# A tuned three-layer kernel: VectorE multiplies each row tile by w_skip, expert scores only of gathered early rows

## The chip, the cores and the metric

The kernel runs on one core of a Trainium2 chip. The metric is the device time of one execution in microseconds (us); the times shown are medians of several executions.

## The reference

Sparse attention over 4 batches of 8 heads (half local, half strided, 576 positions, head size 64), a dense layer pair (512 to 2048 to 512 with a clipped square between), and a mixture of 8 experts behind a skip decision. The last part is what the change touches; `x` holds 2304 rows of 512.

```python
    skip_score = x @ w_skip
    do_compute = skip_score > 0
    out = x.copy()
    xc = x[do_compute]
    logits = xc @ w_gate
    e_idx = np.argmax(logits, axis=1)
    gate_w = softmax(logits)[arange, e_idx]
    for e in range(E):
        mask = e_idx == e
        h = np.maximum(xc[mask] @ w1[e], 0.0)
        y[mask] = gate_w[mask, None] * (h @ w2[e])
    out[do_compute] = xc + y
```

With the inputs that are timed, the reference keeps 4 of the 2304 rows (numbers 11, 23, 1161 and 1177; experts 2, 2, 0 and 2). All others leave as they are.

## The kernel before

The 2304 rows are worked on in 6 chunks (`CHUNKS`) of 384 rows, each of 3 row tiles of 128. A chunk is 16 steps; in step s TensorE forms one 128-wide slice of the hidden layer (`hidden`, L1004, 12 matmuls: each factor is split in a high and a low part, three products of four slices) and adds the slice of two steps earlier to the three row tiles of the output (`output`, L1020, 9 matmuls). In between VectorE clips (L1367) and takes the maximum (L1370), ScalarE squares (L1625) and rounds (L1634), GpSimd forms the low part (L1748). `hidden(s)` waits for the maximum of step s-2; `output` comes two steps after its `hidden`.

All else is hung into 32 places of a chunk (`places_of_chunk`): even places lie, on TensorE, between `hidden` and `output` of a step, odd ones behind `output`; on VectorE even ones lie between clip and maximum, odd ones behind the maximum. Each engine works its own list of jobs in that order, so a job that waits holds everything behind it on its engine. The jobs:

- attention units, one in three places in chunks 2 and 3 (two late ones in chunk 1): `S` scores (PE L829; DVE mask and maximum L1139, L1143; POOL subtracts L1665), `X` exponentials (ACT L1514), `E` sums and reciprocals (DVE L1165 to L1170; POOL scales L1672), `P` transposes (PE L846, ACT L1524), `V` values (PE L865, ACT L1532, DVE L1175).
- `score_jobs(c)`, seven jobs for each chunk c, hung into places 6 to 17 of the chunk behind it: three `Y` (`turn_rows`, PE L875 transposes a row tile, ACT L1540 keeps it), two `Z` (`score_parts`, PE L886 multiplies by w_gate and w_skip), two `A` (`row_scores`, PE L895 adds up groups; DVE L1185 keeps 9 scores a row). For the last chunk they run only in the general part (`PLACES_AFTER`); its skip scores are products of VectorE (`last_skips`, L1312).
- early experts: when the rows of the first 4 chunks are scored, places 19 to 30 of chunk 4 rank all 1536 rows (`rank`, `count` PE L906), find the rows of the first two tiles of 32 slots, each of one expert (`choose` DVE L1259, `info` PE L916, `ids`, `gather` POOL L1700), and load the weights of the first expert (`weights`, SP L747, L750). In chunk 5: `turn`, `first` (PE L932), `back`, `second` (PE L951) for either tile, then the scatter (POOL L1706).
- `left`, `last_skips`: a count of rows still to be computed. Where it is over 0, every engine enters the general part (`for_tiles`), else the kernel ends.

PSUM banks 5 to 7 go round in a ring among all these jobs (`bank_table`); a job waits until the use before it of its bank is read out.

Of the kernel before, what the change touches and what calls it, by code (L numbers as in the profile page):

```python
# [8 lines left out]
F32 = mybir.dt.float32  # L9
# [8 lines left out]
P = 128  # L18
# [114 lines left out]
def places_of_chunk(c):  # L133
# [15 lines left out]
    if c in (2, 3):  # L149
        for i in range(PER_BATCH):  # L150
            unit_at(N_PRO + REST + PER_BATCH * (c - 1) + i, 1 + 3 * i, 4, 5)
    if c == EARLY_CHUNKS:
        for i in range(5):
            got[19 + i].append(("rank", i))
        got[21].append(("count", 0))
        got[25].append(("weights", 0))
        for i in range(2):
            got[24 + i].append(("choose", i))
            got[26 + i].append(("info", i))
            got[27 + i].append(("ids", i))  # L160
            got[28 + i].append(("gather", i))
    if c == EARLY_CHUNKS + 1:
        got[4].append(("skip", 0))
        got[20].append(("left", 0))
        got[4].append(("weights", 1))
        got[9].append(("weights", 2))
        for i in range(2):
            got[i].append(("turn", i))
            got[3 + 11 * i].append(("first", i))
            got[5 + 11 * i].append(("back", i))  # L170
            got[8 + 11 * i].append(("second", i))
    if c > 0:
        for at, job in zip((6, 8, 10, 12, 13, 15, 17), score_jobs(c - 1)):
            got[at].append(job)
# [4 lines left out]
PLACES_AFTER = [score_jobs(CHUNKS - 1)]  # L179


def bank_table():

    n_banks = {"S": 2, "P": 2, "V": 1, "Y": 1, "Z": 1, "A": 1,
               "count": 1, "info": 1, "turn": 1, "first": 1, "back": 1, "second": 1, "total": 1}
# [27 lines left out]
def constants():  # L213
# [20 lines left out]
        "early_restart": np.tile(((np.arange(E * ET) % ET) > 0)[None, :] * 1.0, (P, 1)),  # L234
        "early_edge": np.tile(ES * np.arange(2)[None, :], (P, 1)),
# [13 lines left out]
def build(nc, qk, v, w_in, w_out, w_score_dram, w_skip, w1, w2, out):  # L249
# [4 lines left out]
    with ctx:  # L254
# [33 lines left out]
        y_rows = sb("y_rows", [P, CT, C], F32)  # L288
        y_t = sb("y_t", [P, 2, KT, P], F32)
        steps_end = base[0]  # L290
# [45 lines left out]
        def early(name, hole, shape, dt):  # L336
# [6 lines left out]
                       ["early_slot", "quarter", "early_restart", "early_edge"]]  # L343
        e_table = [early(f"e_table{i}", i, [P, sum(columns[n][2] for n in names)], F32)
                   for i, names in enumerate(early_parts)]
        e_best = early("e_best", 1, [P, ET], F32)
        e_first = early("e_first", 1, [P, ET], F32)
        e_skipped = early("e_skipped", 1, [P, ET], F32)
        e_denom = early("e_denom", 1, [P, ET], F32)
        e_slot = early("e_slot", 1, [P, ET], F32)  # L350
        e_late = early("e_late", 1, [P, ET], F32)
        e_edges = early("e_edges", 1, [P, E, 2], F32)
        e_tiles_of = early("e_tiles_of", 1, [P, E], F32)
        e_tiles_end = early("e_tiles_end", 1, [P, E], F32)
        e_tiles_base = early("e_tiles_base", 0, [P, E], F32)
        e_ended = early("e_ended", 0, [1, 2, E], F32)
        e_expert = early("e_expert", 0, [1, 2], F32)
        e_expert_i = early("e_expert_i", 0, [1, 2], I32)
        e_shifted = early("e_shifted", 2, [P, ET, E], F32)
        e_marks = early("e_marks", 2, [P, ET, E], F32)  # L360
        e_onehot = early("e_onehot", 2, [P, ET, E], F32)
        e_running = early("e_running", 2, [P, E, ET], F32)
        turned_at, hidden_at, hidden_t_at = hole_at[3], hole_at[4], hole_at[5]
        e_chosen = [[early(f"e_chosen{i}{half}", 3 + 2 * i + half, [P, ET // 2, P], BF16) for half in range(2)]
                    for i in range(2)]
        e_values = early("e_values", 7, [P, ET, 6], BF16)
        e_gate_rest = early("e_gate_rest", 7, [P, ET], F32)
        e_info = [early(f"e_info{i}", 7, [P, 8], F32) for i in range(2)]
        e_ids = [early(f"e_ids{i}", 7, [P, 1], U32) for i in range(2)]
        e_rows = [early(f"e_rows{i}", 7, [P, QUART], F32) for i in range(2)]  # L370
        left_of = early("left_of", 0, [P, NT - CT], F32)
# [3 lines left out]

        hole_at[3], hole_at[4], hole_at[5] = turned_at, hidden_at, hidden_t_at
        e_rows_t = [early(f"e_rows_t{i}", 3, [P, P], F32) for i in range(2)]
        e_hidden = early("e_hidden", 4, [P, QF], F32)
        e_hidden_t = early("e_hidden_t", 5, [P, 2, P], F32)
        e_out = [early(f"e_out{i}", 3 + i, [P, QUART], F32) for i in range(2)]  # L380

        w_skip_sb = sb("w_skip_sb", [P, C], F32, offset=x_at + 4 * XR * 6)
        assert 4 * C <= 2 * 4 * CH

        skip_terms = sb("skip_terms", [P, C], F32, offset=attention_at + 4 * KT * FE)
# [93 lines left out]
        e_gates_ready = sem("e_gates_ready")  # L479
# [4 lines left out]
        e_gathered = [sem("e_gathered0"), sem("e_gathered1")]  # L484
# [5 lines left out]
        rows_done = sem("rows_done")  # L490
        left_steps = sem("left_steps")
        skips_ready = sem("skips_ready")
# [152 lines left out]
        def _(sp):  # L645
# [107 lines left out]
            for c in range(CHUNKS):  # L753
                if c == EARLY_CHUNKS:
                    sp.wait_ge(h_full, FT * EARLY_CHUNKS)
                    for i, names in enumerate(early_parts):
                        at = columns[names[0]][0]
                        sp.dma_start(e_table[i][:, :], table_dram[:, at:at + e_table[i].shape[1]])\
                          .then_inc(e_table_loaded, 16)
                for at, jobs in enumerate(PLACES[c]):  # L760
                    for kind, n in jobs:
# [4 lines left out]
                        if kind == "skip":  # L766
                            sp.wait_ge(h_full, FT * (CHUNKS - 1))
                            wait_full(sp, "info", 1)
                            sp.dma_start(w_skip_sb[:, :], w_skip[:, :]).then_inc(w_skip_loaded, 16)
# [4 lines left out]
            def first():  # L774
# [4 lines left out]
                sp.dma_start(r_table[:, :], table_dram[:, first_route:]).then_inc(r_loaded, 16)  # L779

# [26 lines left out]
        def _(pe):  # L807
# [62 lines left out]
            def turn_rows(q):  # L870
                c, t = q // CT, q % CT
                take_bank(pe, "Y", q)
                wait_rows(pe, c, t)
# [25 lines left out]
            def early_counts():  # L899
# [3 lines left out]
                pe.wait_ge(e_step, 6)  # L903
# [6 lines left out]
            def early_info(i):  # L910
                take_bank(pe, "info", i)
                pe.wait_ge(e_placed, 8)
                for t in range(ET):
                    if t % (ET // 2) == 0:
                        pe.wait_ge(e_chosen_ready, 2 * i + 1 + t // (ET // 2))
                    mm = pe.matmul(bank_of("info", i)[:, 0:6], e_chosen[i][t // (ET // 2)][:, t % (ET // 2), :],  # L916
                                   e_values[:, t, :], start=(t == 0), stop=(t == ET - 1))
                mm.then_inc(full_sem("info", i), 1)

            def turn_early_rows(i):  # L920
                take_bank(pe, "turn", i)
                pe.wait_ge(e_gathered[i], 16)
                pe.transpose(bank_of("turn", i)[:, 0:P], e_rows[i][:, :], ident[:, :]).then_inc(full_sem("turn", i), 1)

            def early_first(i):

                take_bank(pe, "first", i)
                wait_free(pe, "turn", i)
                pe.wait_ge(w1_early_loaded, 16 * (i + 1))
                for k in range(KT):  # L930
                    for g in range(4):
                        mm = pe.matmul(bank_of("first", i)[ES * g:ES * (g + 1), 0:QF],  # L932
                                       e_rows_t[i][:, ES * k:ES * (k + 1)], w1_early[:, k, QF * g:QF * (g + 1)],
# [23 lines left out]
            def do_jobs(jobs):  # L957
                for kind, n in jobs:
                    if kind == "count":
                        early_counts()  # L960
                    if kind == "info":
                        early_info(n)
                    if kind == "turn":
                        turn_early_rows(n)
# [107 lines left out]
            def first():  # L1072
# [3 lines left out]
                pe.wait_ge(r_step, 7)  # L1076
# [42 lines left out]
        def _(dve):  # L1119
# [60 lines left out]
            def keep_scores(n):  # L1180
                wait_full(dve, "A", n)
                tiles = score_tiles(n)
                width = E + 1 if n < 2 * (CHUNKS - 1) else E
                rows = bank_of("A", n)[:, 0:SC * len(tiles)].rearrange("p (t e) -> p t e", e=SC)
                dve.tensor_copy(score[:, tiles[0]:tiles[-1] + 1, 0:width], rows[:, :, 0:width])\  # L1185
# [9 lines left out]
            def early_rank(i):  # L1195
                logits, skip = score[:, 0:ET, 0:E], score[:, 0:ET, E]
                per_token = lambda ap: ap.unsqueeze(2).to_broadcast([P, ET, E])
                if i == 0:
                    dve.wait_ge(e_table_loaded, 32)
                    for n in range(2 * EARLY_CHUNKS):  # L1200
                        wait_free(dve, "A", n)
                    early_link(dve.tensor_reduce(e_best[:, :], logits, AX.X, ALU.max))
                    early_link(dve.tensor_tensor(e_shifted[:, :, :], logits, per_token(e_best[:, :]), ALU.subtract))
                order = et("expert_order").unsqueeze(1).to_broadcast([P, ET, E])
                if i == 0:
                    early_link(dve.scalar_tensor_tensor(out=e_marks[:, :, :], in0=e_shifted[:, :, :], scalar=0.0,
                                                        in1=order, op0=ALU.is_equal, op1=ALU.mult))
                if i == 1:
# [649 lines left out]
```

## Time and profile before

| what | us |
|---|---|
| three executions | 528.9, 529.65, 530.3 |
| median | 529.65 |
| the profiled execution, its own time | 529.79 |
| its span, first to last instruction | 527.9 |
| TensorE busy in it | 512.3 |
| VectorE, ScalarE, GpSimd busy | 251.3, 207.2, 211.5 |

The profile is of one execution. Busy time counts an instruction from start to end; matmuls overlap by their pipeline, so what a group of them costs is read from the start of the group to the start of what follows it. A timeline row merges neighbours of one kind (`x4` is four matmuls; a matmul of f32 operands leaves two records). An arrow names the engine and line that ended the wait.

### The profile page before, as it was taken

Reading aid. Unit: us, or ns where it says so; the run is one execution under the profiler, and the core shown is the slowest. Engines: PE = TensorE matmul, PEld = TensorE weight load, DVE = VectorE, ACT = ScalarE, POOL = GpSimd, SP = SyncE. Lnnn points to the kernel's source line nnn. Section 1 sums busy time; section 2 is a strip of 40 time slices with the busy share of each in tenths; the row PEclk is TensorE's granted clock in tenths of the full one; section 3 lists DMA queues with packets and bytes.
Section 4 is the critical chain, followed back from the end, with each engine's and each line's share of the span. In section 5 each row is a group of like instructions: output and inputs, shape, how many; then the busy total and the mean of one; then the engine's idle time right before and its main releaser. Section 6 shows DMA issues by size and latency. Waiting matters only on the chain.

```text
span 527.9 us, 9196 instructions
## 1 busy us (share of the span) xinstructions
PE 512.3 (97%) x3546; PEld 439.2 (83%) x3546; DVE 251.3 (48%) x580; ACT 207.2 (39%) x461; POOL 211.5 (40%) x242
## 2 busy tenths in 40 slices
PE   5899998999999999999999999999999999999996
PEld 3687887889888888888888888888988988887895
DVE  5947657733226435646534646552322483222222
ACT  4956554553332324343433354433232223323122
POOL 0659787662222324544633444542221323221221
PEclk9769999999999999999999999999999999999999
DMA  8992201003001104201210420000300071840001
GB/s 250 343 382 98 70 28 52 31 2 119 1 1 52 64 24 165 76 3 34 91 45 1 166 76 32 2 1 22 115 6 1 0 259 62 299 161 1 2 0 63
DMA packets 19010, 42.22 MB, mean 80 GB/s; under 512 B 2084, under 2 KB 3952, under 8 KB 18964
## 3 DMA queue, kind: packets, MB, share of 16 engines
q1 hardware_dynamic: 18836, 41.59, 22.8%
q8 instruction: 29, 0.48, 0.3%
q14 instruction: 17, 0.14, 0.1%
q0 software_dynamic: 128, 0.02, 0.0%
HBM read 33.06 MB, written 8.78 MB: 79 GB/s over the span
## 4 chain that ended last, share of the span: by engine, by line
PE 88%; DVE 7%; ACT 2%; issue 1%; POOL 1%; DMA 1%; SPq 0%; DVEq 0%; ACTq 0%
PE bank L1004 37%; PE bank L1020 36%; PE bank L865 4%; PE bank L829 4%; PE bank L846 3%; PE bank L875 1%; DVE row_sum L1165 1%; PE bank L886 1%; DVE bank L1148 1%; DVE row_max L1153 1%; DMA qk<-in_qk_dram 1%; DVE prob L1155 1%; PE bank L951 1%; PE bank L932 1%; DVE prob_first L1139 1%
## 5 line engine op out<-in xcount | busy, mean ns | idle before, releaser
L1748 POOL TENSOR_TENSOR g_lo<-act_f,g_hi 128x384 fp32r<-128x384 f32 x96 | 97.1, 1012 | 202.2 <-ACT g_hi L1634 201.9
L1625 ACT ACTIVATE act_f<-act_f,half_col 128x384 f32<-128x384 f32 x96 | 59.2, 616 | 207.4 <-DVE act_f L1367 207.3
L1367 DVE TENSOR_SCALAR act_f<-bank 128x384 f32<-128x384 f32 x96 | 53.2, 554 | 159.7 <-PE bank L1004 155.9
L1004 PE MATMUL bank<-x_hi,win_hi 128*128 128x384 f32 x384 | 90.1, 354 | 0.6 <-DVE act_f L1370 0.6
L1020 PE MATMUL bank<-wout_hi,g_hi 128*128 128x512 f32 x285 | 86.2, 411 | 0.0
L1004 PE MATMUL bank<-x_hi,win_lo 128*128 128x384 f32 x384 | 84.4, 338 | 0.0
L1004 PE MATMUL bank<-x_lo,win_hi 128*128 128x384 f32 x384 | 83.8, 336 | 0.0
L1634 ACT CAST g_hi<-act_f 128x384 fp32r<-128x384 f32 x96 | 49.2, 512 | 84.8 <-DVE act_f L1370 83.9
L1020 PE MATMUL bank<-wout_lo,g_hi 128*128 128x512 f32 x285 | 81.1, 393 | 0.0
L1020 PE MATMUL bank<-wout_hi,g_lo 128*128 128x512 f32 x285 | 80.9, 392 | 0.0
L1004 PEld LDWEIGHTS bank<-x_hi,win_hi 128*128 128x128 f32 x384 | 65.8, 190 | 8.4 <-issue 2.8
L1370 DVE TENSOR_TENSOR act_f<-act_f,bank 128x384 f32<-128x384 f32 x96 | 52.4, 546 | 41.0 <-ACT act_f L1625 39.5
L1004 PEld LDWEIGHTS bank<-x_hi,win_lo 128*128 128x128 f32 x384 | 69.7, 189 | 0.0
L1004 PEld LDWEIGHTS bank<-x_lo,win_hi 128*128 128x128 f32 x384 | 68.7, 189 | 0.0
L1020 PEld LDWEIGHTS bank<-wout_lo,g_hi 128*128 128x128 f32 x285 | 53.5, 188 | 12.6
L1020 PEld LDWEIGHTS bank<-wout_hi,g_lo 128*128 128x128 f32 x285 | 53.5, 188 | 12.2
L1672 POOL TENSOR_TENSOR prob<-prob,row_sum 72x288 f32<-72x288 f32 (+2 forms) x52 | 37.1, 734 | 63.0 <-DVE row_sum L1170 63.0
L1020 PEld LDWEIGHTS bank<-wout_hi,g_hi 128*128 128x128 f32 x285 | 49.0, 188 | 8.6 <-issue 2.5
L1175 DVE TENSOR_TENSOR x_lo<-bank,x_hi 128x288 fp32r<-128x288 f32 (+2 forms) x32 | 18.6, 581 | 42.5 <-ACT x_hi L1532 42.5
L829 PEld LDWEIGHTS bank<-qk 64*96 64x96 f32 (+1 forms) x384 | 18.7, 153 | 10.8 <-issue 7.8
L829 PE MATMUL bank<-qk 64*96 64x128 f32 (+1 forms) x384 | 23.9, 261 | 2.7 <-DMA qk<-in_qk_dram 1.7
L1718 POOL TENSOR_TENSOR wout_lo<-wout_raw,wout_hi 128x512 fp32r<-128x512 f32 x16 | 20.6, 1287 | 12.6 <-ACT wout_hi L1574 12.6
(134 smaller groups left out, 469.2 us busy)
## 6 DMA issues: line engine op xcount, KB each, us to landing
w_early<-in_w_dram SPq DMA_DIRECT2D x4, 2048.0 KB, 8.7
qk<-in_qk_dram SPq DMA_DIRECT2D x12, 592.0 KB, 4.0
out_dram<-y_rows SPq DMA_DIRECT2D x18, 256.0 KB, 2.6
win_raw<-in_w_in_dram SPq DMA_DIRECT2D x16, 256.0 KB, 9.1
wout_raw<-in_w_out_dram SPq DMA_DIRECT2D x16, 256.0 KB, 9.4
y_dram<-y_rows SPq DMA_DIRECT2D x15, 256.0 KB, 2.8
v<-in_v_dram SPq DMA_DIRECT2D x6, 384.0 KB
v<-in_v_dram SPq DMA_DIRECT2D x6, 288.0 KB
```

What stands on the lines that cost most here:

```text
L829: mm = pe.matmul(bank_of("S", n, hh)[0:rows, width * i:width * (i + 1)], buf[head, q_at:q_at + rows], buf[head, k_at:k_at + width], start= ...
L865: mm = pe.matmul(bank_of("V", n)[D * hh:D * hh + D, rows * i:rows * (i + 1)], v_of(u)[0:width, v_at:v_at + D], prob_t_of(u, hh)[:, rows * ...
L1004: mm = pe.matmul(h_ps[s % 2][:, 0:CH], w[:, f, P * k:P * (k + 1)], x[:, k, cols], start=(at == 0), stop=(at == len(order) - 1))
L1020: mm = pe.matmul(y_ps[t][:, :], g[:, s % RING, P * t:P * (t + 1)], w[:, f, :], start=(f == 0 and i == 0), stop=(f == FT - 1 and i == 2))
L1175: dve.tensor_tensor(x_view(x_lo, u), values_view(bank_of("V", n), u), x_view(x_hi, u).bitcast(F32), ALU.subtract).then_inc(free_sem("V", n ...
L1367: dve.tensor_scalar(tile, h_ps[s % 2][:, 0:CH], -1.0, 1.0, ALU.max, ALU.min).then_inc(clip_ready, 1)
L1370: dve.tensor_tensor(tile, tile, h_ps[s % 2][:, 0:CH], ALU.max).then_inc(act_ready, 1)
L1625: act.activation(tile, tile, ACT.Square, bias=half_col[:, 0:1], scale=0.5).then_inc(square_ready, 1)
L1634: act.copy(g_hi[:, s % RING, :], tile).then_inc(g_hi_ready, 1)
L1672: pool.tensor_tensor(tiled(u, hh), tiled(u, hh), over_tiles(u, sums_of(u, hh)), ALU.mult)\
L1718: pool.tensor_tensor(wout_lo[:, f, :], wout_raw[:, f, :], wout_hi[:, f, :].bitcast(F32), ALU.subtract)\
L1748: pool.tensor_tensor(g_lo[:, s % RING, :], act_f[:, s % 2, :], g_hi[:, s % RING, :].bitcast(F32), ALU.subtract).then_inc(g_lo_ready, 1)
```

## The change

- VectorE forms the skip score of each row tile of chunks 0 to 4 by one product with row sum (`row_skip`), from `y_rows` in SBUF and `w_skip_sb` in SBUF, at the even places 6, 10 and 14 of the next chunk (4, 5 and 6 in chunk 4). w_skip is loaded at the start of chunk 1.
- The `Y`, `Z` and `A` jobs leave the chunks. In the general part, if it is entered, all six chunks are scored, the rows of five of them loaded again from DRAM.
- Early experts: the kept rows of the first four chunks are counted by their skip score alone (`flag`, `count`, `slot`, `choose`, `info`, `ids`), up to 32 of them gathered once; their expert scores come from 16 small matmuls (`gate`); `rank`, `present` and `experts` find each row's expert and the two lowest experts present; both experts work on the same 32 slots and each scatters its own rows.
- The general part is entered where more than 32 early rows are kept, where one has a third expert, or where a row of the last two chunks is kept.

The diff, cut to its core:

```diff
-    if c == EARLY_CHUNKS:
-        for i in range(5):
-            got[19 + i].append(("rank", i))
-        got[21].append(("count", 0))
-        got[25].append(("weights", 0))
-        for i in range(2):
-            got[24 + i].append(("choose", i))
-            got[26 + i].append(("info", i))
-            got[27 + i].append(("ids", i))
-            got[28 + i].append(("gather", i))
+    if c > 0:
+        for t, at in enumerate((4, 5, 6) if c == EARLY_CHUNKS else (6, 10, 14)):
+            got[at].append(("skip", CT * (c - 1) + t))
+    if c == EARLY_CHUNKS:
+        for at, kind in ((7, "flag"), (9, "count"), (11, "slot"), (13, "choose"), (15, "info"), (16, "ids"),
+                         (17, "gather"), (20, "turn"), (22, "gate"), (23, "rank"), (25, "present"), (26, "experts"),
+                         (27, "weights")):
+            got[at].append((kind, 0))
     if c == EARLY_CHUNKS + 1:
-        got[4].append(("skip", 0))
...
-            got[i].append(("turn", i))
...
-    if c > 0:
-        for at, job in zip((6, 8, 10, 12, 13, 15, 17), score_jobs(c - 1)):
-            got[at].append(job)
...
-PLACES_AFTER = [score_jobs(CHUNKS - 1)]
+SCORE_ORDER = [CHUNKS - 1] + list(range(CHUNKS - 1))
+PLACES_AFTER = [score_jobs(c) for c in SCORE_ORDER]
...
+                if c == 1:
+                    wait_full(sp, "V", N_PRO - 1)
+                    sp.dma_start(w_skip_sb[:, :], w_skip[:, :]).then_inc(w_skip_loaded, 16)
...
-                by_expert = e_onehot[:, :, :].rearrange("p t e -> p e t")
                 for i, name in enumerate(("ones", "from_here")):
-                    mm = pe.matmul(bank_of("count", 0)[:, E * ET * i:E * ET * (i + 1)]
-                                   .rearrange("p (e t) -> p e t", e=E), et(name), by_expert, start=True, stop=True)
+                    mm = pe.matmul(bank_of("count", 0)[:, ET * i:ET * (i + 1)], et(name), e_flags[:, :],
+                                   start=True, stop=True)
...
+            def early_gates():
+                take_bank(pe, "gate", 0)
+                wait_free(pe, "turn", 0)
+                for k in range(KT):
+                    for g in range(4):
+                        mm = pe.matmul(bank_of("gate", 0)[ES * g:ES * (g + 1), 0:E], e_rows_t[:, ES * k:ES * (k + 1)],
+                                       w_score[:, k, 0:E], start=(k == 0), stop=(k == KT - 1))
...
+            def early_present():
+                take_bank(pe, "present", 0)
+                pe.wait_ge(e_ranked, 2)
+                pe.matmul(bank_of("present", 0)[:, 0:E], et("ones"), e_onehot[:, :], start=True, stop=True)\
+                  .then_inc(full_sem("present", 0), 1)
...
+            def early_experts():
+                wait_full(dve, "present", 0)
+                early_link(dve.scalar_tensor_tensor(out=e_codes[:, :], in0=bank_of("present", 0)[:, 0:E], scalar=0.0,
+                                                    in1=et("expert_order"), op0=ALU.is_gt, op1=ALU.mult))
+                dve.sem_inc(free_sem("present", 0), 1)
+                early_link(dve.tensor_reduce(e_code[:, 0:1], e_codes[:, :], AX.X, ALU.max))
+                early_link(dve.tensor_tensor(e_later[:, :], e_codes[:, :], e_code[:, 0:1].to_broadcast([P, E]),
+                                             ALU.is_lt))
+                early_link(dve.tensor_tensor(e_later[:, :], e_later[:, :], e_codes[:, :], ALU.mult))
+                early_link(dve.tensor_reduce(e_code[:, 1:2], e_later[:, :], AX.X, ALU.max))
+                early_link(dve.tensor_scalar(e_expert[:, :], e_code[0:1, :], -1.0, float(E), ALU.mult, ALU.add))
+                dve.tensor_scalar(e_expert_i[:, :], e_expert[:, :], float(E - 1), None, ALU.min).then_inc(e_routed, 1)
...
+            def row_skip(q):
+                c, t = q // CT, q % CT
+                if q == 0:
+                    dve.wait_ge(w_skip_loaded, 16)
+                wait_rows(dve, c, t)
+                dve.tensor_tensor_reduce(out=skip_terms[:, :], in0=y_rows[:, t, :], in1=w_skip_sb[:, :], scale=1.0,
+                                         scalar=0.0, op0=ALU.mult, op1=ALU.add, accum_out=score[:, q, E:E + 1])\
+                   .then_inc(row_skips, 1)
+                dve.wait_ge(row_skips, q + 1)
...
-                        wait_full(dve, "Y", CT * (c - 1) + t)
+                        dve.wait_ge(row_skips, CT * c)
```

The last pair of lines stands in `keep_sums`, on VectorE and in the same way on ScalarE: what holds a row tile back from being overwritten is now its product, not its transposes.

## Rows read from the trace of the kernel before

**Rows 1.** page: busy time of the engines; granted clock in 40 slices

```profile
PE 512.3 (97%) x3546; PEld 439.2 (83%) x3546; DVE 251.3 (48%) x580; ACT 207.2 (39%) x461; POOL 211.5 (40%) x242
PEclk9769999999999999999999999999999999999999
```

**Rows 2.** waits of TensorE, whole span: us in total, times, longest us

```profile
PE bank L846 <- POOL prob L1672: 0.3, 2, 0.2
```

**Rows 3.** groups of instructions; busy us, mean ns of one

```profile
L875 PE MATMUL bank<-ident,y_rows 128*128 128x128 f32 x60 | 9.3, 277 | 0.0
L886 PE MATMUL bank<-y_t,w_score 128*32 128x256 f32 (+1 forms) x80 | 5.3, 338 | 0.0
L895 PE MATMUL bank<-add_groups,y_t 128*128 128x9 f32 x30 | 4.2, 238 | 0.0
```

**Rows 4.** timeline, TensorE, chunk 1; start us, us, engine, line

```profile
124.51 0.87 PE L1004 MATMUL bank<-x_hi,win_hi 128*128 128x384 f32 x4
128.69 0.87 PE L1004 MATMUL bank<-x_hi,win_hi 128*128 128x384 f32 x4
...
156.99 0.94 PE L1004 MATMUL bank<-x_hi,win_hi 128*128 128x384 f32 x4
```

**Rows 5.** timeline, TensorE, chunk 4

```profile
381.17 0.87 PE L1004 MATMUL bank<-x_hi,win_hi 128*128 128x384 f32 x4
...
413.71 0.87 PE L1004 MATMUL bank<-x_hi,win_hi 128*128 128x384 f32 x4
...
426.97 0.87 PE L1004 MATMUL bank<-x_hi,win_hi 128*128 128x384 f32 x4
...
436.11 0.87 PE L1004 MATMUL bank<-x_hi,win_hi 128*128 128x384 f32 x4
```

**Rows 6.** timeline, TensorE, chunk 2, a transpose group behind the values of a unit

```profile
208.61 0.72 PE L865 MATMUL bank<-prob_t,v 72*64 72x72 f32 x16
209.26 0.66 PE L875 MATMUL bank<-ident,y_rows 128*128 128x128 f32 x4
209.67 0.93 PE L1020 MATMUL bank<-wout_hi,g_hi 128*128 128x512 f32 x3
```

**Rows 7.** timeline, all engines, chunk 2: from one unit's values to the next one's transposes

```profile
217.90 0.72 PE L865 MATMUL bank<-prob_t,v 72*64 72x72 f32 x16
218.72 0.70 ACT L1532 CAST x_hi<-bank 128x288 fp32r<-128x288 f32 x1 [0.37 <-PE bank L865]
219.46 0.72 DVE L1175 TENSOR_TENSOR x_lo<-bank,x_hi 128x288 fp32r<-128x288 f32 x1 [2.66 <-ACT x_hi L1532]
220.33 0.81 DVE L1165 TENSOR_REDUCE row_sum<-prob 72x4 f32<-72x288 f32 x2 [0.15 <-DVE x_lo L1175]
221.51 0.64 PE L886 MATMUL bank<-y_t,w_score 128*32 128x256 f32 x8
221.65 1.29 POOL L1672 TENSOR_TENSOR prob<-prob,row_sum 72x288 f32<-72x288 f32 x2 [2.21 <-DVE row_sum L1170]
222.08 0.96 PE L1020 MATMUL bank<-wout_hi,g_hi 128*128 128x512 f32 x3
224.25 0.66 PE L846 MATMUL bank<-ident,prob 72*72 72x72 f32 x8
```

**Rows 8.** chain that ended last, the second expert product; start us, us, engine, line

```profile
462.22 1.89 PE bank L951 x64
```

**Rows 9.** groups: the row products of the last chunk; busy us, mean ns

```profile
L1312 DVE CUSTOM_DVE_ANT_0 skip_terms<-bank,w_skip_sb 128x512 f32<-128x512 f32 x3 | 2.1, 691 | 3.2 <-PE bank L1033 3.1
```

**Rows 10.** timeline, chunk 4: VectorE beside GpSimd

```profile
424.08 0.26 DVE L1245 SCALAR_TENSOR_TENSOR e_running<-e_tiles_base,e_running 128x96 f32<-128x96 f32 x1
424.20 1.02 POOL L1748 TENSOR_TENSOR g_lo<-act_f,g_hi 128x384 fp32r<-128x384 f32 x1 [2.73 <-ACT g_hi L1634]
424.38 1.06 DVE L1248 TENSOR_TENSOR e_running<-e_running,e_onehot 128x96 f32<-128x96 f32 x1
```

**Rows 11.** DMA issues; KB each, median us from issue to landing

```profile
w_early<-in_w_dram SPq DMA_DIRECT2D x4, 2048.0 KB, 8.7
```

More of the change, by code:

```diff
@@ L171, in places_of_chunk @@
             got[8 + 11 * i].append(("second", i))
-    if c > 0:
-        for at, job in zip((6, 8, 10, 12, 13, 15, 17), score_jobs(c - 1)):
-            got[at].append(job)
     return got
 PLACES = [places_of_chunk(c) for c in range(CHUNKS)]
-PLACES_AFTER = [score_jobs(CHUNKS - 1)]
+SCORE_ORDER = [CHUNKS - 1] + list(range(CHUNKS - 1))
+PLACES_AFTER = [score_jobs(c) for c in SCORE_ORDER]
 def bank_table():
     n_banks = {"S": 2, "P": 2, "V": 1, "Y": 1, "Z": 1, "A": 1,
-               "count": 1, "info": 1, "turn": 1, "first": 1, "back": 1, "second": 1, "total": 1}
+               "count": 1, "info": 1, "turn": 1, "gate": 1, "present": 1, "first": 1, "back": 1, "second": 1,
+               "total": 1}
     used = [0] * 8
@@ L342, in build @@
         early_parts = [["from_here", "ones", "expert_order", "token_high", "token_low"],
-                       ["early_slot", "quarter", "early_restart", "early_edge"]]
+                       ["early_slot", "quarter"]]
         e_table = [early(f"e_table{i}", i, [P, sum(columns[n][2] for n in names)], F32)
                    for i, names in enumerate(early_parts)]
[L346 to L371, printed above, removed]
+        left_of = early("left_of", 0, [P, CT + 2], F32)
         left_flags = early("left_flags", 0, [P, CT + 1], BF16)
@@ L917, in early_info, with turn_early_rows @@
                                    e_values[:, t, :], start=(t == 0), stop=(t == ET - 1))
[L918 to L923, printed above, removed]
+                mm.then_inc(full_sem("info", 0), 1)
+            def turn_early_rows():
+                take_bank(pe, "turn", 0)
+                pe.wait_ge(e_gathered, 16)
+                pe.transpose(bank_of("turn", 0)[:, 0:P], e_rows[:, :], ident[:, :]).then_inc(full_sem("turn", 0), 1)
@@ L961, in do_jobs @@
                     if kind == "info":
-                        early_info(n)
+                        early_info()
                     if kind == "turn":
-                        turn_early_rows(n)
+                        turn_early_rows()
+                    if kind == "gate":
+                        early_gates()
+                    if kind == "present":
+                        early_present()
                     if kind == "first":
@@ L1256, in early_choose @@
+            def early_choose():
                 shape = [P, ET // 2, P]
@@ L1271, in early_ids, with early_row_ids @@
+            def early_row_ids():
+                wait_full(dve, "info", 0)
+                dve.tensor_copy(e_info[:, 0:4], bank_of("info", 0)[:, 0:4]).then_inc(e_info_steps, 1)
+                dve.wait_ge(e_info_steps, 1)
+                dve.sem_inc(free_sem("info", 0), 1)
+                dve.tensor_scalar(e_info[:, 4:5], e_info[:, 2:3], -4.0 * N, 4.0 * N, ALU.mult, ALU.add)\
                    .then_inc(e_info_steps, 1)
-                dve.scalar_tensor_tensor(out=mine[:, 1:2], in0=mine[:, 0:1], scalar=64.0, in1=mine[:, 1:2],
+                dve.scalar_tensor_tensor(out=e_info[:, 1:2], in0=e_info[:, 0:1], scalar=64.0, in1=e_info[:, 1:2],
@@ L1420, in first @@
                 dve.wait_ge(r_loaded, 16)
-                for n in range(2 * (CHUNKS - 1), 2 * CHUNKS):
+                for n in range(2 * CHUNKS):
                     wait_free(dve, "A", n)
@@ L1781, in first @@
                 pool.wait_ge(y_kept, 16 * CT)
+                for i in range(2):
+                    pool.wait_ge(e_scattered[i], 16)
                 for i in range(2):
```

316 lines of the change are left out of this document (158 added, 158 removed).

## The prediction, made before the changed kernel was run

> **What bounds the kernel now.** First the page: TensorE is busy for 512.3 of 527.9 us, no other engine for half of them, and its granted clock stands at nine tenths or more in nearly every slice, the upper of its two levels, 2.4 GHz [rows 1]. So TensorE sets the time, and what matters is what its list holds and where it waits. The view of its waits says how near the other engines are: in the whole span it waits for the scaled probabilities of an attention unit twice, 0.3 us in all [rows 2]. That is small but not slack: at those two places, the last units of chunks 2 and 3, the chain of the other engines ends just when TensorE comes. Durations of single matmuls overlap, so I price a TensorE job by the start of what follows it, and a plain step is 128.69 - 124.51 = 4.18 us [rows 4].
>
> **Terms that TensorE loses.** The Y, Z and A groups add up to 9.3 + 5.3 + 4.2 = 18.8 us of busy time [rows 3]; the timeline shows what they cost.
> - Chunk 1 has them among plain steps: 156.99 - 128.69 = 28.30 for six steps that would take 25.1, so 3.2 us. Chunk 4 gives the same: 413.71 - 381.17 = 32.54 less 7 x 4.18 = 3.3 [rows 4, 5]. Chunk 5 holds the same seven jobs. Three chunks x 3.2 = 9.6 us.
> - In chunks 2 and 3 attention jobs stand beside them, and part of the hand-over is paid anyway. A Y behind V costs 209.67 - 209.26 = 0.41 [rows 6], the first Z 222.08 - 221.51 = 0.57 [rows 7]. For the second Z and the two A, whose groups are smaller, I take 0.9 in all (estimate, from busy means of 0.34 and 0.24 a record in pairs and fours [rows 3]). 3 x 0.41 + 0.57 + 0.9 = 2.7 a chunk, 5.4 us for two.
> - Sum: 15.0 us, with bounds of 14 and 16.
>
> **The early part, on TensorE.** The count with 96 columns costs 426.97 - 413.71 - 3 x 4.18 = 0.7; with 12 columns I take 0.4, near the A jobs of 9 columns: -0.3. Two info jobs cost 436.11 - 426.97 - 2 x 4.18 = 0.8; one goes: -0.4. One of two turns goes, a single transpose: -0.15. The new `gate` is 16 matmuls of the shape of `second` (weights of 32 columns, four groups side by side) with 8 columns moving: 32 records. The nearest row is `second` itself, 64 records in 1.89 us, 0.03 each [rows 8]: 0.95 and 0.1 of hand-over. Bounds: 0.5 if a record of 8 columns is half of one of 128, 2.3 at the 0.57 / 8 of the Z group [rows 7]. `present` is half a count: +0.35. Net +0.55 us, from 0 to 1.8.
>
> **What VectorE gains and who pays.** A row product took 0.69 us [rows 9], one operand read from PSUM; with both in SBUF I take 0.74 with the read of the sum. Fifteen are added, 11 us on an engine that is idle for half of the span; the keeping of A's scores goes. In chunks 1, 4 and 5 a product lies between clip and maximum, where VectorE waits for ScalarE's square anyway; `hidden(s)` needs the maximum of step s-2, a whole step (over 4 us) after the clip, so they cost nothing. Behind the product on VectorE are queued the maximum and the next place's jobs; behind the maximum, ScalarE's rounding.
>
> In chunks 2 and 3 that is not free. The local chain is: values V of one unit leave TensorE (217.90), ScalarE rounds (218.72), VectorE forms the rest (219.46) and the sums of the next unit (220.33), GpSimd scales (221.65 + 1.29 = 222.94), TensorE transposes (224.25, second head about 0.25 later) [rows 7]. Slack 1.5 us. The change takes work out of exactly this gap: Z's 0.57 here and about 0.2 of hand-over, 0.4 to 0.8 in its neighbours. So 0.5 to 0.8 us is left at units 1 to 4 of each chunk; the last unit has none [rows 2]. Into that comes the product. At place 6 it stands ahead of the maximum of its step and of the masking of the next unit; ScalarE's list is in order, so exponentials and rounding of V wait behind the later `g_hi`. Followed, the rounding of V starts some 0.8 us later against V than before, at places 10 and 14 again, less what ScalarE wins by losing the 15 copies of Y. I get waits of TensorE of 0 at unit 2, 0.1 to 0.8 at unit 3, 0.2 to 0.9 at unit 4: 0.9 a chunk, 1.8 us for two, bounds 0 and 5 (below).
>
> The trace shows that VectorE and GpSimd can hold each other up: a product of two SBUF tiles of 96 columns took 1.06 us and ended 0.2 behind the GpSimd subtraction that had begun 0.18 before it, where one of the same size just ahead of that subtraction took 0.26 [rows 10]. A row product has both operands in SBUF, and at places 6 and 10 it is issued just when GpSimd starts to scale or shift a unit. By the Trainium skill, page "SBUF — State Buffer", section "Who interferes with whom", a VectorE instruction with two SBUF inputs and a GpSimd instruction that reads SBUF share a read interface, and the second one blocks for the whole of the first. The trace agrees in that row; what it would make of the time is rival 2.
>
> **Moved steps.** The load of w_skip goes from chunk 5 to the head of chunk 1 on SP's queue, ahead of the qk and v loads of chunk 2; its wait (values of unit 5) is long past, and it has six places, 12 us, to land: nothing. The stores of a chunk no longer wait on transposes but on products: earlier. In chunk 4 the experts are known at place 26 instead of 22, so the first weights (4 MB) are issued later by nearly 5 places. `first` of chunk 5 comes 8 half steps after place 27, over 15 us; the landing took 8.7 us at the median [rows 11]. Nothing; it would take 6 us more to cost one. The gather (place 17) to `turn` (place 20) is three half steps, 6 us. On GpSimd the gather now stands behind ids of place 16; behind it only the next `g_lo`, which has two steps.
>
> **The sum.** 15.0 - 0.55 - 1.8 = 12.65 us off the profiled execution's 529.79, which is 517.1. The median of the three executions is 0.14 below the profiled one: 517.0.
>
> **Rivals.**
> 1. The cover holds: no new waits in chunks 2 and 3. Then 15.0 - 0.55 = 14.45: 515.2. For it: slack never goes under 0.5 except at the last unit, where nothing is removed. Against: my hand count of the shift of ScalarE's rounding.
> 2. The lock on the SBUF read: products at places 6 and 10 are held for a whole scale or shift of both heads (1.29 us [rows 7]), or hold GpSimd up. Six products in two chunks x 0.5 to 1.3 of extra delay, of which the slack of 0.5 absorbs a part: 3 us of waits on top: 520.0. For it: rows 10. Against: VectorE mostly comes first at place 6, and then GpSimd loses only 0.7.
> 3. Slower: the general part is entered. Its price is the seven scoring jobs of six chunks, 6 x 3.2 = 19 us, and a tile on top, with at least the 4 MB of weights (8.7 us) and their use: over 30 us, 545 or more. It decides from one row: a kept row of the last two chunks, a third expert, or a 33rd early row. The inputs give 4 rows, all in the first four chunks, of two experts, so only a fault of the count would do it.
> 4. The gates or a late load of weights cost more than thought (2.3 us for `gate`): 518.5; inside the range.
>
> **How the numbers follow.** The forecast (516.0 to 518.8) 0.45; rival 1 with down to 514.3 0.27; rival 2 0.20; rival 3 0.02; others, between 520.5 and 528, 0.06. The range takes in the forecast, both of the first rivals, and the bounds of the sum: 514.2 to 520.5. A difference under 0.3% is about what a measurement of this kernel can tell from no change. Faster by more than that 0.97, within it 0.01, slower 0.02.
>
> **What would show it.** Right: no rows of L875, L886, L895 at all; chunk 4's steps at 4.18 us between early jobs; a `gate` group of about 1 us; waits of TensorE for GpSimd's scaling of 1 to 3 us in chunks 2 and 3, where before they were 0.3. Rival 1: these stay under 0.6. Rival 2: row products over 1 us at places 6 and 10, or GpSimd's scaling beside them lengthened, and waits over 4 us. Wrong altogether: a TensorE wait for `w_early`, for the gathered rows, or for the maximum L1370, or instructions behind `left_i`.

## The result

The changed kernel takes 513.61 us (median of four executions, 513.08 to 514.7), the kernel before 529.61 beside it. The ratio is 0.970 (95% interval 0.968 to 0.972): 3% faster, 16.0 us. A second set on another occasion gave 513.58 us and 0.971 (0.969 to 0.972). The prediction was 517.0 with a range from 514.2 to 520.5: the way was right, and the gain was larger than the range allowed for.

The profiled execution took 513.08 us, its span is 511.3. From the page of the changed kernel, the line that answers to the first of [rows 1]: TensorE is as full as before, 97% of the span, and has 16.4 us less to do; VectorE has 6 us more, ScalarE 10 us less (251.3 and 207.2 in [rows 1]).

```profile
PE 495.9 (97%) x3397; PEld 427.3 (84%) x3397; DVE 257.5 (50%) x594; ACT 196.8 (38%) x435; POOL 211.9 (41%) x235
```

TensorE's waits in the changed kernel (us in total, times, longest), against [rows 2]: the wait for scaled probabilities is 0.4 us where it was 0.3. No wait for weights of the early experts, for gathered rows or for a row product appears; the 0.6 us for the maximum (L1409) are as before (0.6 at L1370).

```profile
PE bank L844 <- DVEq L1179: 1.8, 2, 1.5
PE bank L1024 <- DVE act_f L1409: 0.6, 2, 0.4
PE bank L844 <- POOL prob L1710: 0.4, 2, 0.2
```

Where did the time go? The chunks tell it, measured from the first group of `hidden` of one chunk to that of the next (the last one to the group of its last step). Windows cut at these points show chunks 1 and 2 of the kernel before, then of the changed one; columns: stretch, length, busy time and instructions of each engine (TensorE, its weight loads, VectorE, ScalarE, GpSimd), granted clock, DMA share, GB/s.

```profile
116.05:191.55 75.50, 75.23 (x433) 65.88 (x431) 29.18 (x59) 24.14 (x49) 19.74 (x21) 1.00 0.14 46
191.55:280.08 88.53, 88.36 (x651) 75.16 (x650) 46.29 (x108) 34.78 (x79) 38.98 (x48) 1.00 0.18 62
```

```profile
114.51:186.77 72.26, 72.00 (x398) 63.88 (x397) 30.76 (x63) 22.07 (x44) 19.79 (x21) 1.00 0.14 48
186.77:272.60 85.83, 85.65 (x618) 72.94 (x616) 48.91 (x112) 32.86 (x74) 40.17 (x48) 1.00 0.19 64
```

| stretch | before | changed | less | predicted |
|---|---|---|---|---|
| up to chunk 1 | 116.05 | 114.51 | 1.54 | 0 |
| chunk 1 | 75.50 | 72.26 | 3.24 | 3.2 |
| chunk 2 | 88.53 | 85.83 | 2.70 | 1.8 |
| chunk 3 | 88.53 | 85.82 | 2.71 | 1.8 |
| chunk 4 | 71.69 | 68.71 | 2.98 | 2.5 |
| chunk 5, to its last step | 74.91 | 71.51 | 3.40 | 3.35 |

The five chunks give 15.03 us. They repeat: in further executions of either program, and in the experiments that leave a chunk alone, each chunk has the same length within 0.04 us. The 1.54 us ahead of chunk 1 are another matter (below); behind the last step of chunk 5 the two programs differ by 0.1 us.

In chunk 2 the chain of [rows 7] in the changed kernel, rows of the timeline of all engines:

```profile
212.36 0.72 PE L863 MATMUL bank<-prob_t,v 72*64 72x72 f32 x16
213.18 0.70 ACT L1570 CAST x_hi<-bank 128x288 fp32r<-128x288 f32 x1
213.91 0.72 DVE L1195 TENSOR_TENSOR x_lo<-bank,x_hi 128x288 fp32r<-128x288 f32 x1 [1.74 <-ACT x_hi L1570]
214.78 0.81 DVE L1185 TENSOR_REDUCE row_sum<-prob 72x4 f32<-72x288 f32 x2 [0.15 <-DVE x_lo L1195]
216.11 1.29 POOL L1710 TENSOR_TENSOR prob<-prob,row_sum 72x288 f32<-72x288 f32 x2 [1.78 <-DVE row_sum L1190]
218.18 0.66 PE L844 MATMUL bank<-ident,prob 72*72 72x72 f32 x8
```

The rounding begins 213.18 - 212.36 = 0.82 us after V, exactly as before (218.72 - 217.90). The scaled probabilities are ready at 217.40, TensorE comes at 218.18: 0.8 us are left of the 1.3 before (224.25 - 222.94).

### The profile page after: what moved, and what is told of

The parts are those of the page before. It is cut to its first block, busy times and chain, and to the rows that moved or that the text cites. A ratio compares the mean times of both kernels' runs of the same rounds, so it can differ in the third digit from the quotient of the medians.

```text
span 511.3 us, 8844 instructions
## 1 busy us (share of the span) xinstructions
PE 495.9 (97%) x3397; PEld 427.3 (84%) x3397; DVE 257.5 (50%) x594; ACT 196.8 (38%) x435; POOL 211.9 (41%) x235
## 4 chain that ended last, share of the span: by engine, by line
PE 87%; DVE 8%; ACT 2%; issue 1%; POOL 1%; DMA 1%; SPq 0%; DVEq 0%; ACTq 0%
PE bank L1024 37%; PE bank L1040 37%; PE bank L863 4%; PE bank L827 3%; PE bank L844 3%; DVE row_sum L1185 1%; DVE prob_first L1159 1%; DVE bank L1168 1%; DVE row_max L1163 1%; DMA mask_l<-shape_constants 1%; DVE row_max L1173 1%; DVE prob L1175 1%; PE bank L967 1%; PE bank L948 1%; POOL prob L1710 1%
## 5 line engine op out<-in xcount | busy, mean ns | idle before, releaser
L1409 DVE TENSOR_TENSOR act_f<-act_f,bank 128x384 f32<-128x384 f32 x96 | 52.5, 547 | 37.0 <-ACT act_f L1663 34.2
L1703 POOL TENSOR_TENSOR prob<-prob,row_max 72x288 f32<-72x288 f32 (+1 forms) x32 | 24.7, 790 | 4.0 <-DVE row_max L1163 4.0
```

The source lines that it names most:

```text
L1409: dve.tensor_tensor(tile, tile, h_ps[s % 2][:, 0:CH], ALU.max).then_inc(act_ready, 1)
L1703: pool.tensor_tensor(tiled(u, hh), tiled(u, hh), over_tiles(u, peak_of(u, hh)), ALU.add)\
```

## The experiments

All of them start from the changed kernel, except the copy of the kernel before. Chunks are compared with 72.26, 85.83, 85.82, 68.71 and 71.51 us.

**1. No products in chunks 2 and 3.**

```diff
+                if CT <= q < 3 * CT:
+                    dve.memset(score[:, q, E:E + 1], -1.0).then_inc(row_skips, 1)
+                    dve.wait_ge(row_skips, q + 1)
+                    return
```

A memset of one column (0.06 us) marks the rows as not kept in place of the product.

> The changed kernel without the six row products that VectorE makes in chunks 2 and 3 (rows 384 to 1151 are marked as not kept instead; no kept row lies there). Theory 'the cover holds': products there cost TensorE nothing, so chunks 2 and 3 stay at 85.83 and 85.82 us from first hidden group to first hidden group, TensorE's waits for GpSimd's scaling stay at 0.4 us in all, the time within 0.5 us of the changed kernel's 513.6. Theory 'they cost something after all, and the seven score jobs gave more than was reckoned': both chunks get shorter by 0.3 to 0.9 us each.

Chunks 2 and 3: 85.83 and 85.82 us. The time of 515.06 us (2 executions) misses the half microsecond that was expected, with chunk 1 starting at 116.64, 2.1 us later than in the changed kernel; the chunks behind it are the same. So the products cost TensorE nothing at all, and the 2.7 us a chunk are the whole price of the score jobs there, as summed.

**2. Three products for each one.**

```diff
-                dve.tensor_tensor_reduce(out=skip_terms[:, :], in0=y_rows[:, t, :], in1=w_skip_sb[:, :], scale=1.0,
...
+                times = 3 if CT <= q < 3 * CT else 1
+                for _ in range(times):
+                    row_products[0] += 1
+                    dve.tensor_tensor_reduce(out=skip_terms[:, :], in0=y_rows[:, t, :], in1=w_skip_sb[:, :],
+                                             scale=1.0, scalar=0.0, op0=ALU.mult, op1=ALU.add,
+                                             accum_out=score[:, q, E:E + 1]).then_inc(row_steps, 1)
+                    dve.wait_ge(row_steps, row_products[0])
```

> Each of the six row products of chunks 2 and 3 is made three times, one behind the other (1.5 us more of VectorE at each of places 6, 10 and 14). 'The cover holds, but is thin' (0.6 to 1.0 us of slack left at the transposes of units 2 to 4, read off the trace): TensorE now waits, 0.3 to 1.0 us at three units of a chunk, chunks 2 and 3 longer by 1 to 3 us each. 'VectorE is off the path altogether there': under 0.2 us each.

Chunk 2: 90.59 us (+4.8), chunk 3: 91.76 (+5.9, of which 1.2 with a lower clock, see the last section), 525.12 us (8 executions, 523.29 to 528.13), 0.993 of the kernel before (0.990 to 0.996). This is more than the 1 to 3 us a chunk that the thin cover was said to cost, and it comes by two steps that the expectation did not name. TensorE's waits:

```profile
PE bank L864 <- ACT prob_t L1569: 3.6, 3, 1.7
PE bank L845 <- DVE prob L1160: 3.3, 2, 1.6
PE bank L845 <- POOL prob L1717: 1.2, 5, 0.3
```

The timeline of chunk 2 there shows both (selected rows): masking of the next unit (L1160) is queued behind the products on VectorE, and the second half of the transposes needs the PSUM bank that it reads; later ScalarE's copy of the transposes (L1569) stands in its list behind a rounding (L1679) that waited for the maximum (L1416) behind the products.

```profile
212.56 0.81 DVE L1160 SCALAR_TENSOR_TENSOR prob<-bank,mask_s 72x288 f32<-72x288 f32 x2
213.06 0.45 PE L845 MATMUL bank<-ident,prob 72*72 72x72 f32 x4 [1.65 <-DVE prob L1160]
...
224.39 0.56 DVE L1416 TENSOR_TENSOR act_f<-act_f,bank 128x384 f32<-128x384 f32 x1
224.98 0.51 ACT L1679 CAST g_hi<-act_f 128x384 fp32r<-128x384 f32 x1 [4.28 <-DVE act_f L1416]
225.40 0.69 ACT L1569 COPY prob_t<-bank 72x288 f32<-72x288 f32 x2
226.23 0.72 PE L864 MATMUL bank<-prob_t,v 72*64 72x72 f32 x16 [1.67 <-ACT prob_t L1569]
```

**3. Products behind the attention units.**

```diff
-        for t, at in enumerate((4, 5, 6) if c == EARLY_CHUNKS else (6, 10, 14)):
+        for t, at in enumerate((4, 5, 6) if c == EARLY_CHUNKS else (6, 10, 14) if c > EARLY_CHUNKS else (28, 29, 30)):
```

> The products of chunks 1 to 3 are moved from places 6, 10, 14 to 28, 29, 30, behind all attention units. The shared read of SBUF: products back at 0.68 us each, no GpSimd pair of scaling or shifting over 1.61 us, where now one pair takes 2.03 and one 1.63 instead of 1.29 and two products take 1.80. If the collisions cost TensorE nothing, chunks 2 and 3 keep 85.8 us; if they did, both get shorter by up to 0.5 us.

Chunks 2 and 3: 85.83 and 85.82 us; 514.46 us (2 executions). The edit moves the products of chunk 1 too, which takes 72.28 us. No product or GpSimd instruction of chunks 2 and 3 is lengthened any more, and no time goes with it. First the changed kernel, then this one, groups between 188 and 300 us (busy us, mean ns of one):

```profile
L1703 POOL TENSOR_TENSOR prob<-prob,row_max 72x288 f32<-72x288 f32 x14 | 9.8, 716 | 2.2 <-DVE row_max L1163 2.2
L1312 DVE CUSTOM_DVE_ANT_0 skip_terms<-y_rows,w_skip_sb 128x512 f32<-128x512 f32 x4 | 3.8, 938 | 0.0
```

```profile
L1703 POOL TENSOR_TENSOR prob<-prob,row_max 72x288 f32<-72x288 f32 x14 | 9.0, 664 | 2.2 <-DVE row_max L1163 2.2
L1312 DVE CUSTOM_DVE_ANT_0 skip_terms<-y_rows,w_skip_sb 128x512 f32<-128x512 f32 x4 | 2.7, 682 | 0.0
```

**4. The kernel before, once more.** No edit.

> The kernel before, once more, to see how its start varies. The changed kernel reached chunk 1 at 114.51 us and this one at 116.05, though their work up to there is the same; the granted clock of 30 to 40 us was 0.89 against 0.74. 'Chance of the execution': this copy starts chunk 1 anywhere from 114.5 to 116.1, and over several profiles both programs show both. 'The change does it': again 116.0, while copies of the changed kernel stay at 114.5. Chunks 1 to 4 in either case 75.50, 88.53, 88.53, 71.69 us within 0.1.

Chunk 1 started at 115.76 us, the chunks took 75.49, 88.56, 88.54, 71.68 us; 530.0 us (8 executions, 528.82 to 530.24). The start lies near that of the first profile and within both expectations, so this run alone does not decide between them (see "The start" below).

**5. Two products for each one.** As experiment 2, with `times = 2`.

> Each of the six row products of chunks 2 and 3 made twice (0.75 us more of VectorE at each place). With one product a chunk takes 85.83 us, with three 90.59. 'There is a threshold': slack of 0.6 to 1.0 us at units 2 to 4 takes in most of the second product; chunk 2 longer by 0 to 1 us. 'Every microsecond of VectorE there costs the same from the first on': half of what three cost, 88.2 us.

Chunks 2 and 3: 87.73 us each, +1.9; 519.67 us (one execution; 0.8 us of it lie behind the last step of chunk 5, where the edit does nothing). One product costs 0, two 1.9, three 4.8 a chunk: a threshold, but it lies nearer than expected, inside the second product. The waits are the same two kinds, 0.6 us at a time:

```profile
PE bank L864 <- ACT prob_t L1569: 1.8, 4, 0.6
PE bank L845 <- DVE prob L1160: 1.2, 2, 0.6
```

**6. The gate job five times.**

```diff
-                for k in range(KT):
+                for k in [k for _ in range(4) for k in range(KT)] + list(range(KT)):
```

> The 16 matmuls of the gate job are made five times (four times 32 records more of 128x32 weights with 8 columns). By the prediction's price of 0.03 us a record chunk 4 grows by 3.8 us; by what the changed kernel's timeline shows for the group (0.37 us for 32 records, 0.012 each) by 1.5 us, from 68.71 to 70.2 us. All other chunks unchanged.

Chunk 4: 69.77 us, +1.06 for 128 records, 0.008 each (515.3 us, one execution). The price of 0.03 was too high by a factor of more than three, and even the 0.012 read from the group's own length was above it. The timeline of TensorE in the changed kernel shows the single job, 408.01 - 407.64 = 0.37 us:

```profile
407.64 0.44 PE L931 MATMUL bank<-w_score,e_rows_t 128*32 128x8 f32 x32
408.01 0.97 PE L1040 MATMUL bank<-wout_hi,g_hi 128*128 128x512 f32 x3
```

**7. GpSimd subtracts from unit 13 on.**

```diff
-                if n < N_PRO or u.b >= 2:
+                if n < N_PRO or n >= 13:
...
-                    if kind == "S" and UNITS[n].b >= 2:
+                    if kind == "S" and n >= 13:
```

> From attention unit 13 on (the last of chunk 0 and the two in chunk 1) the scores are masked into SBUF and GpSimd subtracts the maximum, as it does for batches 2 and 3; PSUM banks come free after the mask. The waits of TensorE for the bank that VectorE frees after its subtraction (1.8 us in two places, 1.5 in chunk 0 and 0.3 in chunk 1) should go: chunk 1 0.3 us shorter, start of chunk 1 1.5 us earlier than in copies with the same clock, 1.0 to 1.8 us off in all. Rival: in chunk 0 GpSimd is busy for most of the time (w_in and w_out rests), the subtraction comes late there and the wait only changes its name: 0 or slower.

513.19 us (5 executions), 0.9685 of the kernel before (0.967 to 0.970); the changed kernel beside it took 513.58 (experiment 8). Chunk 1 got shorter by 0.5 us (71.77), but the wait in chunk 0 stayed: the bank belonged to unit 12, one earlier than I had counted.

```profile
93.11 0.45 PE L844 MATMUL bank<-ident,prob 72*72 72x72 f32 x4 [1.52 <-DVEq L1179]
```

**8. The changed kernel, once more.** No edit.

> The changed kernel once more, on the same chip as the two beside it. Chunks 72.26, 85.83, 85.82, 68.71 us within 0.1; start of chunk 1 anywhere from 114.5 to 116.6 us; time 513.5 to 515, ratio to the kernel before 0.970 to 0.973.

513.58 us (5 executions, 513.2 to 514.74), start of chunk 1 at 114.54, chunks 72.27, 85.86, 85.81, 68.71.

**9. GpSimd subtracts from unit 12 on.** As experiment 7, with 12 in both places.

> As pool_shift_13, but from unit 12 on. The trace of pool_shift_13 still shows one wait of 1.5 us for the bank that VectorE frees after its subtraction, at a transpose in chunk 0: that bank belongs to unit 12. Chunk 1 stays at 71.77 us, this wait goes: 1.5 us off pool_shift_13's 513.2, so 511.7, ratio 0.966. Rival: GpSimd's weight rests fill its list at that place, the exponentials of unit 12 come later and another wait takes the place: no gain.

512.33 us (5 executions, 511.93 to 512.75), 0.968 of the kernel before (0.966 to 0.970). That is the lowest time of all, though 0.6 above the 511.7 expected. Against the changed kernel's 513.58 it is 1.3 us less, but that was another occasion, on which the kernel before took 0.5 us more (529.54 against 529.02), and the intervals of the two ratios touch (0.969 to 0.972 there). What the trace shows is that chunk 1 takes 71.77 us as in experiment 7, and that the wait of 1.8 us is gone. In the windows of the end of chunk 0, first the changed kernel, then this one, TensorE goes from 34.46 us busy of 36 to 36.00:

```profile
80.00:116.00 36.00, 34.46 (x245) 29.77 (x244) 21.78 (x42) 19.63 (x43) 25.07 (x24) 1.00 0.07 20
```

```profile
80.00:116.00 36.00, 36.00 (x255) 31.39 (x254) 21.74 (x41) 19.77 (x43) 28.96 (x29) 1.00 0.10 31
```

**10. Products ahead of the last unit.**

```diff
-        for t, at in enumerate((4, 5, 6) if c == EARLY_CHUNKS else (6, 10, 14)):
+        for t, at in enumerate((4, 5, 6) if c == EARLY_CHUNKS else (21, 22, 23) if c in (2, 3) else (6, 10, 14)):
```

> The six products of chunks 2 and 3 at places 21, 22, 23, ahead of the last unit's sums, where TensorE already waits 0.2 us a chunk (no slack). 'A product is free only where slack covers it': chunks 2 and 3 0.4 to 1.5 us longer than 85.83. 'VectorE has time enough anywhere': within 0.1.

Chunks 2 and 3: 86.29 and 86.28 us, +0.46 each; 514.94 us (one execution). The wait is not where I looked for it (the last unit's probabilities), but at the V of the unit before it, again for ScalarE's copy:

```profile
PE bank L863 <- ACT prob_t L1562: 1.0, 2, 0.5
```

**11. ScalarE gets its copies back.**

```diff
+    if c in (2, 3):
+        for at, n in ((6, 512), (8, 512), (10, 256), (13, 512), (15, 128)):
+            got[at].append(("copy", n))
...
+                        act.copy(act_scratch[:, 0:n], w_skip_sb[:, 0:n]).then_inc(act_copied, 1)
+                        act.wait_ge(act_copied, act_copies[0])
```

> ScalarE gets back work of the size and at the places of the copies that the change took from it in chunks 2 and 3 (512, 512, 256, 512 and 128 columns at places 6, 8, 10, 13, 15), product kept. 'Losing these copies is what paid for the products': TensorE waits of 0.2 to 0.9 us appear at units 2 to 4, chunks 2 and 3 0.4 to 2 us longer. 'The products fitted into slack as it was': chunks 85.8 us as before.

Chunks 2 and 3: 85.92 and 85.96 us, +0.1; 515.01 us (one execution). The copies write another type but take as long (0.6 us for 512 columns). The chain in chunk 2 moves, though TensorE hardly does:

```profile
214.05 0.72 PE L868 MATMUL bank<-prob_t,v 72*64 72x72 f32 x16
215.48 0.70 ACT L1575 CAST x_hi<-bank 128x288 fp32r<-128x288 f32 x1
218.40 1.29 POOL L1723 TENSOR_TENSOR prob<-prob,row_sum 72x288 f32<-72x288 f32 x2 [1.74 <-DVE row_sum L1195]
219.86 0.66 PE L849 MATMUL bank<-ident,prob 72*72 72x72 f32 x8
```

The rounding now begins 215.48 - 214.05 = 1.43 us after V instead of 0.82, so 0.6 later, and of the 0.8 us ahead of the transposes 219.86 - 219.69 = 0.17 are left. So the missing copy did keep the delay away from the rounding; with the copy back, the slack at the transposes takes nearly all of it in.

## Why the prediction failed

- **What bounds the kernel, and the terms that TensorE loses:** right. 3.2 us a chunk among plain steps (measured 3.24), 2.7 beside attention jobs (2.70 and 2.71). 15.0 us was the sum, and the starts of groups priced it; the 18.8 us of busy time in [rows 3] would not have.
- **New waits in chunks 2 and 3, 1.8 us:** this is the step that failed. Experiment 1 shows 0. The error stands in "Followed, the rounding of V starts some 0.8 us later against V than before": it started at the same 0.82. The product does push VectorE's list back. The rows below, of the kernel before, of the changed kernel and of experiment 3 (which has no product there), are read against the start of V: 217.90, 212.36 and 214.48.

```profile
212.58 0.50 DVE L1370 TENSOR_TENSOR act_f<-act_f,bank 128x384 f32<-128x384 f32 x1
215.00 0.56 DVE L1367 TENSOR_SCALAR act_f<-bank 128x384 f32<-128x384 f32 x1 [0.47 <-PE bank L1004]
217.36 0.57 ACT L1540 COPY y_t<-bank 128x512 f32<-128x512 f32 x1
217.83 0.52 ACT L1634 CAST g_hi<-act_f 128x384 fp32r<-128x384 f32 x1
```

```profile
208.46 0.56 DVE L1409 TENSOR_TENSOR act_f<-act_f,bank 128x384 f32<-128x384 f32 x1
210.38 0.55 DVE L1406 TENSOR_SCALAR act_f<-bank 128x384 f32<-128x384 f32 x1
212.74 0.50 ACT L1672 CAST g_hi<-act_f 128x384 fp32r<-128x384 f32 x1
```

```profile
209.91 0.50 DVE L1409 TENSOR_TENSOR act_f<-act_f,bank 128x384 f32<-128x384 f32 x1
214.31 0.50 ACT L1672 CAST g_hi<-act_f 128x384 fp32r<-128x384 f32 x1
214.48 0.72 PE L863 MATMUL bank<-prob_t,v 72*64 72x72 f32 x16
215.30 0.69 ACT L1570 CAST x_hi<-bank 128x288 fp32r<-128x288 f32 x1 [0.49 <-PE bank L863]
```

  The maximum began 5.32 us ahead of V before, 4.57 in experiment 3 and 3.90 in the changed kernel. So it came 0.75 us later against V because TensorE, with less in its list, reaches V sooner, and 0.67 later by the product. The first shift was taken in by the idle time of the clip (0.47 before, none in experiment 3 or the changed kernel) and by ScalarE's missing copy (0.57). The product's shift still stood at 0.55 on ScalarE's `g_hi` (0.17 ahead of V in experiment 3, 0.38 behind it in the changed kernel). Next in that list is the rounding of V, and in experiment 3 ScalarE idled 0.49 us there until V came; in the changed kernel it no longer idles, and begins the rounding at the same 0.82. So the 0.8 us ahead of the transposes were not touched. After the product at place 14 it is the same: the rounding begins 0.85 us behind V. The prediction had added up the delays on the way, had taken little or nothing off for the missing copy (its 0.8 is near the 0.6 that experiment 11 shows with the copy in place), and had set only the slack at TensorE's end of the chain against them, not the idle time at the rounding.
- **The mechanism itself** was a real one. Experiments 5, 2 and 10 show it at 1.9, 4.8 and 0.5 us a chunk, by ScalarE's list order as the prediction said, and by the bank of the next unit's mask, which it named only as queued. One product lies just under the threshold; by experiment 5 less than one more product fits.
- **Rival 1, the cover holds:** this is what happened. Its 515.2 us were 0.6 above what the chunks alone give, 529.65 - 15.03 = 514.6; most of that is the early part. It had 0.27 where it deserved the largest share. 514.6 lies inside the stated range: what took the measured time below it are the last 1.0 us, nearly all of them ahead of chunk 1 ("The start"), which no term of the prediction dealt with.
- **Rival 2, the shared read of SBUF:** the collisions came, the cost did not. In the changed kernel a product issued 0.35 us behind a GpSimd shift took 1.80 us instead of 0.68, and a shift overtaken by a product took 2.03 for the pair instead of 1.29:

```profile
217.63 2.03 POOL L1703 TENSOR_TENSOR prob<-prob,row_max 72x288 f32<-72x288 f32 x2 [0.24 <-DVE row_max L1163]
217.83 0.68 DVE L1312 CUSTOM_DVE_ANT_0 skip_terms<-y_rows,w_skip_sb 128x512 f32<-128x512 f32 x1
...
227.27 1.61 POOL L1703 TENSOR_TENSOR prob<-prob,row_max 96x384 f32<-96x384 f32 x2
227.62 1.80 DVE L1312 CUSTOM_DVE_ANT_0 skip_terms<-y_rows,w_skip_sb 128x512 f32<-128x512 f32 x1
```

  By the rule of the Trainium skill (page "SBUF — State Buffer", section "Who interferes with whom") the second of the two is blocked. The pair at 227.27 agrees: the product came second and was held. The pair at 217.63 does not by its start times: the shift began 0.20 us ahead of the product, yet the product took its plain 0.68 and the shift was lengthened. So the traces show that the two hold each other up, and not that it is always the later one. Experiment 3 removes every such collision and gains 0.00 us, so here it never reaches TensorE. It hit hardest at place 14, where the prediction had not looked. At place 6 it came near: the scaling beside the product took 1.63 us instead of 1.29 and ended at 209.57, and TensorE began the transposes at 209.63.

```profile
207.94 1.63 POOL L1710 TENSOR_TENSOR prob<-prob,row_sum 72x288 f32<-72x288 f32 x2 [5.23 <-DVE row_sum L1190]
```

- **The early part, +0.55 us:** mis-sized, it is +0.1. With the score jobs of chunks 4 and 5 at 3.24 + 3.2 (an estimate from chunk 1, as measured and as read before), the two chunks got shorter by 2.98 + 3.40. The term that failed is `gate`: 0.37 us and its hand-over instead of 1.05, with 0.27 us for its 32 records by experiment 6, below the lower bound of 0.5. A record with 8 columns moving is far from half of one with 128.
- **Moved steps:** right; nothing waited for weights, gather or w_skip.
- **The start:** of the 16.0 us between the medians, 15.0 are in the chunks and 0.1 behind the last step; by subtraction 0.9 lies ahead of chunk 1 and was in no term. In the two profiled executions it is 1.54. The work up to there is the same; the windows of 30 to 40 us, first of before, then of the changed kernel, show the granted clock at 0.74 and 0.89 of full speed: TensorE stayed at the lower of its two levels for longer in the one.

```profile
30.00:40.00 10.00, 9.62 (x53) 8.40 (x51) 5.79 (x13) 4.68 (x10) 5.87 (x5) 0.74 1.04 383
```

```profile
30.00:40.00 10.00, 9.63 (x57) 8.71 (x56) 6.97 (x18) 5.93 (x12) 6.80 (x7) 0.89 1.05 387
```

  Over the profiles of experiments 1 to 6, 8, 10 and 11, whose work up to there is the same too, chunk 1 starts between 114.5 and 116.6 us, and executions of one program lie up to 2.3 us apart (528.1 to 530.4 for the kernel before). That is 0.4% of the time, more than the 0.3% that the prediction took for what a measurement can tell. Both programs know the early start: from the spans of single executions less the constant stretch behind the start of chunk 1 (an estimate: 527.9 - 116.05 = 411.85 before, 396.8 changed), the kernel before begins chunk 1 anywhere from 114.4 to 116.8 (spans of 526.2 to 528.6) and the changed kernel from 114.5 to 116.1 (511.3 to 512.9). Whether the changed program tends to the early start (both of its own profiles have 114.5, its variants 115.4 to 116.6) is open; what the change itself is shown to give is 15.0 us.

## What to carry to other kernels

Work put on an engine off the critical path is paid first from the idle time in front of each later instruction of the chain that follows it, and only then from the slack where the chain ends. Read the bracket of each instruction on the way, take the added time off one after the other, and only the rest is a wait. Read these brackets with the rest of the change in place, best in a copy without the added work: here the largest idle time of the kernel before (0.47 us) was gone already when the product came, and 0.49 us elsewhere took it in. Price a job on the bounding engine from the start of its group to the start of what follows. And do not read "hidden" as "free to add more": here one product of 0.7 us cost nothing and a second one cost 1.9 us a chunk, because two lists and a bank were late together.

## What the runs showed of the hardware

- Small matmuls with weights of 32 columns in four groups side by side cost 0.008 us a record at 8 columns (experiment 6), against 0.03 at 128 columns [rows 8]. A record is half a matmul here: 16 matmuls leave 32.
- In experiment 2, TensorE waited 1.65 us in chunk 3, as it had in chunk 2; but this time the granted clock fell after it (mean 0.83 over 300 to 310 us), and chunk 3 took 1.2 us more than chunk 2 with the same work. So the stretch behind a wait of TensorE can cost more than the wait. That the wait brought the clock down is inferred from the order alone: chunk 2 with the same wait, and a second wait of 1.65 us in chunk 3 itself (it ended at 318 us), kept full clock. What decides between them stays open.

```profile
300.00:310.00 10.00, 8.35 (x54) 6.83 (x53) 6.20 (x14) 3.48 (x8) 5.21 (x6) 0.83 0.05 13
```
